# Causal attention followed by a gated MLP on one core: five batches of attention output turned on TensorE instead of three, and filling matmuls that count twice in the time of the planner

## The reference, cut to what matters

```python
scores = q @ k.T / 8, masked where block_i < block_j (blocks of 64 positions)
attn   = softmax(scores); attn_out = attn @ v        # [8, 8, 576, 64]
x      = attn_out.transpose(0, 2, 1, 3).reshape(4608, 512)
h      = x @ w_in                                    # 512 -> 2048
out    = (h / (1 + exp(-beta * h))) @ w_out          # 2048 -> 512, float32
```

## Time and profile before

| | us |
|---|---|
| median of three runs | 356.59 |
| the profiled execution's own time | 356.37 |
| its span, first to last instruction | 354.6 |
| TensorE busy (matmuls) | 326.8 |
| VectorE, ScalarE, GpSimd busy | 220.0, 211.2, 81.9 |

### The profile page before, as it was taken

The page is one execution under the profiler, slowest core; times in us unless marked ns, Lnnn a source line. Parts: engine busy times, 40 slices in busy tenths (PEclk is TensorE's granted clock), DMA queues, the critical chain, the costliest instruction groups (busy, mean ns, idle before and its releaser), DMA issues.

```text
span 354.6 us, 7475 instructions
## 1 busy us (share of the span) xinstructions
PE 326.8 (92%) x3103; PEld 205.4 (58%) x3081; DVE 220.0 (62%) x447; ACT 211.2 (60%) x314; POOL 81.9 (23%) x127
## 2 busy tenths in 40 slices
PE   7898999999989999779986699999799999999995
PEld 5574464445765467434653456665566666666684
DVE  4648783697745875257763276686358757756742
ACT  1937962487648866558855178747585545545521
POOL 6684272115314303330034103510300000000000
PEclk9999999999999999998999699999999999999999
DMA  7999899989999986778679979798322020020023
GB/s 212 218 250 229 180 229 233 216 181 218 215 178 259 203 162 160 172 128 159 142 145 191 176 167 204 161 191 150 83 59 65 2 89 31 0 91 30 0 92 118
DMA packets 112673, 53.08 MB, mean 150 GB/s; under 512 B 82928, under 2 KB 112128, under 8 KB 112640
## 3 DMA queue, kind: packets, MB, share of 16 engines
q1 hardware_dynamic: 97792, 38.82, 55.1%
q10 hardware_dynamic: 9280, 9.44, 8.2%
q0 software_dynamic: 5568, 4.36, 7.8%
HBM read 36.71 MB, written 9.44 MB: 130 GB/s over the span
## 4 chain that ended last, share of the span: by engine, by line
PE 54%; DMA 15%; SPq 6%; ACT 4%; issue 3%; DVE 2%; POOL 2%; ACTq 1%; POOLq 0%
PE PS L952 23%; PE PS L882 19%; PE PS L736 5%; DMA w_out<-in_moe_w_out_dram 4%; DMA ST<-in_k_dram 4%; PE PS L684 4%; SPq L768 3%; DMA ST<-in_q_dram 3%; PE PS L988 3%; ACT E L698 2%; DMA QKT<-QKn 2%; POOL QKn L645 2%; ACT th L962 1%; DMA xT<-xq 1%; DVE gT L966 1%
## 5 line engine op out<-in xcount | busy, mean ns | idle before, releaser
L962 ACT ACTIVATE th<-PS,beta 128x512 f32<-128x512 f32 x144 | 96.9, 695 | 73.3 <-PE PS L952 73.0
L952 PE MATMUL PS<-xT,w_in 128*128 128x512 bf16 x542 | 133.3, 385 | 5.5 <-POOL QKn L645 2.0
L966 DVE SCALAR_TENSOR_TENSOR gT<-th,PS 128x512 f16<-128x512 f32 x144 | 96.2, 683 | 41.2 <-ACT th L962 40.8
L698 ACT ACTIVATE E<-PS 128x1024 bf16<-128x1024 f32 x93 | 92.1, 1030 | 34.9 <-PE PS L684 34.3
L952 PEld LDWEIGHTS PS<-xT,w_in 128*128 128x128 bf16 x576 | 53.7, 99 | 60.2 <-issue 5.1
L882 PE MATMUL PS<-w_out,gT 128*128 128x256 f16 x512 | 64.2, 273 | 0.5 <-ACT ost L897 0.5
L882 PEld LDWEIGHTS PS<-w_out,gT 128*128 128x128 f16 x512 | 48.4, 98 | 12.7 <-issue 1.1
L645 POOL CAST QKn<-ST 128x640 bf16<-128x640 f32 x48 | 35.8, 746 | 48.6 <-DMA ST<-in_k_dram 26.6
L736 PE MATMUL PS<-Vn,E 128*128 128x65 bf16 x930 | 33.6, 195 | 13.0 <-DMA xT<-xq 6.1
L559 POOL CAST Vn<-Vs 128x640 bf16<-128x640 f32 (+1 forms) x28 | 19.9, 710 | 109.6 <-DMA Vs<-in_v_dram 108.4
L736 PEld LDWEIGHTS PS<-Vn,E 128*128 128x128 bf16 x930 | 32.0, 99 | 18.8 <-DMA xT<-xq 6.9
(11 more groups left out here) (60 smaller groups left out, 179.1 us busy)
## 6 DMA issues: line engine op xcount, KB each, us to landing
out_dram<-ost ACTq DMA_DIRECT2D x36, 256.0 KB, 2.5
Vs<-in_v_dram SPq DMA_DIRECT2D x24, 256.0 KB, 4.7
ST<-in_q_dram SPq DMA_DIRECT2D x8, 288.0 KB, 6.0
ST<-in_k_dram SPq DMA_DIRECT2D x8, 288.0 KB, 6.6
w_in<-in_moe_w_in_dram POOLq DMA_DIRECT2D x4, 512.0 KB, 11.5
w_out<-in_moe_w_out_dram POOLq DMA_DIRECT2D x4, 512.0 KB, 12.3
OV<-in_v_dram SPq DMA_DIRECT2D x4, 256.0 KB, 11.2
Vs<-in_v_dram SPq DMA_DIRECT2D x6, 128.0 KB, 8.0
```

Source lines behind the costliest of these rows:

```text
L698: return g.activation(E3[es_(te)][:, g0, :, :], PS[:, ps.slot:ps.slot + 2, :], ACT.Exp, scale=0.125)
L952: z = g.matmul(PS[:, ph.slot, :], w_in[:, c, 128 * j:128 * j + 128], xT[:, c, row % RX:row % RX + RC], start=(c == 0), stop=(c == 3))
L962: return g.activation(th[tt.slot][:], PS[:, ph.slot, :], ACT.Tanh, scale=beta[:, j:j + 1])
L966: return g.scalar_tensor_tensor(out=gT[tg.slot][:, j, :], in0=th[tt.slot][:], scalar=1.0, in1=PS[:, ph.slot, :], op0=ALU.add, op1=ALU.mult)
```

## The change

Two numbers change. XB goes from 3 to 5, so that the eight units of batches 3 and 4 are turned by TensorE and VectorE as those of batches 0 to 2 were. And all fills after the first twelve are booked at 220 ns instead of 110. The matmuls of a fill stay as they are. 40 fills stand in the program where 66 stood.

```diff
-        QB, XB, CAST = 2, 3, "POOL"
+        QB, XB, CAST = 2, 5, "POOL"
...
-            n = 215 if i < 12 else 110
+            n = 215 if i < 12 else 220
```

## The result

Four executions of the changed kernel took 341.17 to 342.50 us, median 341.85. Four of the kernel before on the same chip had a median of 356.48. The ratio is 0.9616 (95% interval 0.9551 to 0.9681): about 14 us faster. Forecast was 346.0 with a range of 339 to 357. The profiled execution took 342.35 us, with a span of 340.5.

A forecast was written before the change was run, and what follows sets the result against it. The prediction took TensorE's work plus its waits, mainly at 140 to 210 us, as the bound. 356.37 − 7.4 − 7.7 + 3.7 + 1.0 − 0.3 = 345.7, with 0.2 for the median 346 us; range 339 to 357.

The forecast's parts named there:

- rival 3: More goes than counted: the 1.7 us of idle from 210 to 260 us, and part of the transposes hides; 341 us, chance 0.12.
- Waits of batches 3 and 4, and of batch 5: TensorE's waits and low clock at 140 to 210 us all go: −7.4 us for batches 3 and 4, −7.66 for batch 5.
- the five waits: TensorE, 140 to 210 us, 11.82 us: first for unit 15, third for V, second, fourth and fifth for `xq` buffers.
- TensorE's new work: 40 transposing matmuls for eight units, 0.46 us a unit, all on the path: +3.7 us, bounds 0 and 8.8.
- rival 4: The transposing matmuls on TensorE don't overlap: 8.8 instead of 3.7 us, 351 us in all, chance 0.03.
- VectorE's new work: 20 copies of 0.301 us, 6.0 us, hidden in VectorE's idle time at 140 to 210 us: no cost.
- The new wait: TensorE's transposes wait for `xq`, mostly covered; bank and order waits add +1.0 us in 140 to 210 us.
- What was counted as staying: TensorE's 3.13 us of idle from 210 to 260 us; its reduction to 1.4 was not in the forecast's sum.
- Fills: In front of the first scores, six fills instead of 11 let scores start earlier: −0.3 us, bounds −0.8 and 0.
- rival 2: The clock falls in the first 30 us, as half the fills are gone: 347 to 349 us, chance 0.10.
- Rival 1: Batch 5 still waits, as its transposes meet the load of q of batch 7: 353.4 us, chance 0.17.
- Rival 5: The waits are the loads' own and move to later batches, so none goes: slower, 360.8 us, chance 0.08.

## Why the prediction was right

The chain of causes that the forecast rests on came, but the time is that of rival 3: 341.85 us is nearer to its 341 than to 346. Of rival 3 one half holds, the idle time that goes from 210 to 260 us; the other doesn't, since the turning hides in nothing. From unit 11 on the sum gave 5.25 us too little gain, and the front then lost 1.55; that these cancel in part is luck.

- **Waits of batches 3 and 4, and of batch 5.** Right: the five waits are gone, and with them the lower clock of that stretch. The run with a third buffer shows that the second, fourth and fifth are waits for an `xq` buffer, and the runs with plain copies and with halves that the issues of the transposes in SP's list made them.
- **TensorE's new work.** Right in kind, slightly too high: 3.11 us on the timeline, where 3.7 was taken from one unit of batch 2, the longest of its four (the other three take 0.33 us). Running it twice adds 2.8 to 3.2 us, so it lies on the path. That excludes rival 4.
- **VectorE's new work.** Counted at nothing, and no wait for it shows: with 20 more copies TensorE idles less than before.
- **The new wait.** The +1.0 for bank and order waits had the wrong sign. I allowed 2.0 us of idle in 140 to 210 us; 0.85 is left.
- **What was counted as staying.** The 3.13 us of idle from 210 to 260 us fell to 0.58, more than rival 3 allowed. K of batch 6 goes out 24 us earlier, and no wait over 0.3 us is left there.

From unit 11 to the end the forecast was −7.4 − 7.7 + 3.7 + 1.0 = −10.4 us, and the traces show −15.65. The windows from unit 11 to the end, of before and then of the changed kernel:

```profile
102.36:354.60 252.24, 232.03 (x2112) 149.58 (x2099) 152.90 (x295) 148.92 (x222) 38.01 (x52) 0.98 0.57 123
```
```profile
103.91:340.50 236.59, 230.65 (x2151) 150.74 (x2139) 157.63 (x315) 148.69 (x222) 39.49 (x52) 1.00 0.58 125
```

TensorE's idle time fell from 20.21 to 5.94 us, by 14.27. Its busy time fell by 1.38 although 3.11 came in, so its other work got 4.49 us shorter. Of that, 3.26 is the low clock that the prediction read; the remaining 1.2 I can't assign to rows.

- **Fills.** The forecast of −0.3 holds for nothing that can be measured: with XB 3 the ratio is 1.0008, and with XB 5 the fills booked as before give 341.47 against 341.85. The scores do start 0.80 us earlier, but V is late, and the profiled front lost 1.55 us. That is the mechanism of rival 2, in this execution, and about its price: at the lower clock the 60 multiplications alone take 1.50 us longer. Its time of 347 to 349 didn't come, since the other terms gave more. Of the four executions one was granted 1.00 on the whole and was the longest, 342.50 us, so the fall doesn't explain the differences between them. What lands V later there and what makes the clock fall I couldn't settle.
- **Rival 1** was half right: unit 20's transposes are held by the load of q. The hold is 6.16 us and costs nothing.
- **Rival 5** was wrong in its sum and right in one point: the length of the holds is the loads'. With them in another queue SP's holds are gone, while the transposes next to a load still land with it.

**The step that failed is a reason, not a term.** I wrote: "it was SP's order that put a small transpose behind a large load". By that, anything at that place would wait as long. Plain copies at the same places, in the same order, took the five waits away. Two half copies each brought four of the five back, and the whole time with them. So the place is one half. The other is how many issues stand there, and how long each holds SP: 0.60 us for a copy of any of the two sizes and 1.24 us for a transpose when the queue is free, and several times as much behind a load. Everything behind them on SP starts later by that sum, and after a few units the next large load too. The Trainium skill's "Advanced Engine Details and Errata", section "X-Bar Transpose (TRN2)", by which transposing DMAs are as fast as regular ones, agrees with the landing here (2.6 against 2.4 us) and not with the issue (1.24 against 0.60 us). By the median landing alone the copies would have changed next to nothing.

The 390 ns of the Trainium skill's "VectorE: DVE Perf Modes", section "The three transpose paths", would have made the new matmuls cost 15.6 us. Five of them in a row take 0.39 us here.

## What to carry to other kernels

Where one engine issues all transfers in order, count its issues and what each holds, not only bytes and landing times: a small DMA behind a large load holds everything that comes after it. Work that leaves such a list can be worth doing on the engine that bounds the kernel, if it costs that engine less (here 3.1 us) than the waits that the list makes (here 14.3 us of idle time and 3.3 of low clock). Read idle time by stretch, and ask of each wait which list it comes from; a further buffer takes away the waits for that buffer (349.77 us here), a shorter list takes all that hang on it (341.85).

## What the runs showed of the hardware

A plain DMA from `xq` to `xT` held SP for 0.60 us whether it moved 128 or 64 partitions, and a crossbar transpose there for 1.24 us; behind a load of q or k the same issues took up to 4.97 us (copies), 5.12 (halves) and 7.45 (transposes). With the loads issued by ScalarE a transpose held SP for 2.36 us at most, but those issued next to a load still took up to 8.2 us to land, together with the load. Five transposing matmuls in a row take 0.33 to 0.47 us of TensorE's time in batches 3 and 4, although each is listed with 0.219 us. With each fill run twice, TensorE was granted half its clock for 4 us in which it was busy without a gap, after a stretch in which it was busy for 3.21 of 4 us; other kernels with 3.32 and 3.62 us there kept the full clock, so these records alone don't say when it falls or rises.
